# Top-32 attention, gated feed-forward and mixture of experts: the head mask as marks by ScalarE and one GpSimd subtraction, row norm and value product on GpSimd

## What is computed

```
B, H, S, D = 2, 8, 576, 64
scores = q @ k.T / sqrt(D)                       # per head, 576 x 576
keep the 32 largest of each row, the rest -> -1e9
attn = exp(scores - max); attn /= sum + 1e-9
x = (attn @ v) as 1152 rows of 512

xn  = x / sqrt(mean(x*x) + 1e-6) * rms_g
x   = (silu(xn @ w_gate) * (xn @ w_val)) @ w_out     # 512 -> 1536 -> 512

e   = argmax(x @ r_gate), gate = its softmax probability      # 8 experts, room for 288 rows each
out = gate * (relu(x @ w1[e]) @ w2[e])                        # 512 -> 1024 -> 512
```

## Time and profile before

| | |
|---|---|
| median of 3 runs | 741.94 us (741.75 to 743.79) |
| span of the profiled execution, first to last instruction | 741.7 us (the runs list no separate time for it; the median lies 0.2 us above the span) |
| PE busy | 686.1 us, 93% |
| DVE busy | 478.9 us, 65% |
| ACT busy | 270.4 us, 36% |
| POOL busy | 281.5 us, 38% |
| mean granted TensorE clock | 0.948 |

### The profile page before, as it was taken

How to read it: one execution, slowest core, us unless ns; L and a number is a source line. 1 busy time by engine, 2 the same in 40 slices (tenths; PEclk the granted TensorE clock), 3 DMA queues, 4 the chain that set the end, 5 groups by cost and what they waited for, 6 DMA issues and landing times.

```text
span 741.7 us, 10642 instructions
## 1 busy us (share of the span) xinstructions
PE 686.1 (93%) x3862; PEld 557.7 (75%) x3862; DVE 478.9 (65%) x1090; ACT 270.4 (36%) x545; POOL 281.5 (38%) x233
## 2 busy tenths in 40 slices
PE   5696789999999999999999999999994999999994
PEld 3574667588687578688688688687653999999994
DVE  3999979989979968979979979972211011111110
ACT  4385565354354354354354354342210011101110
POOL 1556665646455445545546455452000011110002
PEclk9666599999999999999999999999995999999998
DMA  9999000000000000000000000000055677676501
GB/s 186 363 384 263 0 15 1 0 15 1 14 15 1 15 15 1 11 20 1 14 15 1 15 1 0 15 2 15 0 212 166 256 263 259 231 245 234 204 20 34
DMA packets 52908, 65.43 MB, mean 88 GB/s; under 512 B 32058, under 2 KB 32058, under 8 KB 52860
## 3 DMA queue, kind: packets, MB, share of 16 engines
q1 hardware_dynamic: 51116, 60.05, 25.3%
q0 software_dynamic: 1744, 4.76, 1.7%
HBM read 52.89 MB, written 12.30 MB: 88 GB/s over the span
## 4 chain that ended last, share of the span: by engine, by line
PE 81%; DVE 13%; ACT 1%; DMA 1%; issue 1%; POOL 1%; SPq 0%; POOLq 0%; DVEq 0%; ACTq 0%
PE ps L451 13%; PE ps L593 10%; PE ps L607 10%; PE ps L423 10%; PE ps L401 8%; PE ps L440 6%; PE ps L444 6%; PE ps L441 6%; PE ps L414 4%; PE ps L388 3%; DVE w_top L1006 3%; DVE m L1001 3%; DVE w_parts L909 2%; DVE w_top L993 2%; DVE m L982 1%
## 5 line engine op out<-in xcount | busy, mean ns | idle before, releaser
L1116 POOL TENSOR_SCALAR s_ring<-s_ring,m 128x576 f32<-128x576 f32 x72 | 124.3, 1727 | 179.4 <-DVE m L1010 148.2
L423 PEld LDWEIGHTS ps<-arena,pt_ring 128*128 128x128 f32 (+3 forms) x800 | 99.9, 187 | 22.9 <-issue 8.9
L423 PE MATMUL ps<-arena,pt_ring 128*128 128x65 f32 (+3 forms) x800 | 107.6, 274 | 3.8 <-ACT pt_ring L666 3.7
L1006 DVE MATCH_REPLACE8 w_top<-m,w_top 128x576 f32<-128x576 f32 x144 | 105.8, 742 | 0.0
L1118 POOL TENSOR_TENSOR p_ring<-p_ring,s_ring 128x576 f32<-128x576 f32 x72 | 102.0, 1417 | 6.0
L1001 DVE MAX8 m<-w_top 128x8 f32<-128x576 f32 x144 | 101.6, 747 | 0.0
L451 PE MATMUL ps<-wo_space,hid 128*128 128x512 f32 x216 | 95.8, 593 | 0.0
L401 PE MATMUL ps<-arena,q_cols 128*128 128x288 f32 (+1 forms) x320 | 92.4, 444 | 2.1 <-ACT q_cols L666 1.4
L440 PE MATMUL ps<-w_parts,x_hi 128*128 128x512 f32 x216 | 92.3, 428 | 0.9 <-ACT x_hi L666 0.8
L666 ACT ACTIVATE pt_ring<-ps 128x512 f32<-128x512 f32 (+1 forms) x144 | 54.0, 428 | 95.9 <-PE ps L415 95.6
L441 PE MATMUL ps<-w_parts,x_hi 128*128 128x512 f32 x216 | 85.2, 395 | 0.0
(11 more groups left out here) (116 smaller groups left out, 812.1 us busy)
## 6 DMA issues: line engine op xcount, KB each, us to landing
w_loads<-in_moe_w SPq DMA_DIRECT2D x16, 2048.0 KB, 9.0
dispatched_rows<-hid SPq DMA_DIRECT2D x18, 260.0 KB, 7.4
w_loads<-in_moe_w_gate SPq DMA_DIRECT2D x1, 3072.0 KB, 10.8
w_loads<-in_moe_w_val SPq DMA_DIRECT2D x1, 3072.0 KB, 18.6
wo_space<-in_moe_w_out SPq DMA_DIRECT2D x1, 3072.0 KB, 13.6
arena<-dispatched_rows SPq DMA_DIRECT2D x8, 341.2 KB
out_rows<-hid SPq DMA_DIRECT2D x9, 256.0 KB, 5.2
q_space<-in_q SPq DMA_DIRECT2D x8, 256.0 KB, 2.9
```

Source lines behind the costliest of these rows:

```text
L423: last = mm(ao_ps(u % H, r0, r1), pt_ring[0:n, u % 2, j * P + r0:j * P + r1], vs[b][0:n, j, u % H, :], start=(j == 0), stop=(j == KC - 1))
L1006: vec.match_replace(w_top[:, a, :], m8[:, u % 8, i, :], w_top[:, a, :], NEG).then_inc(s["top_step"], 1)
L1116: gp.tensor_scalar(sc, sc, m8[:, n % 8, TOPK // 8 - 1, 7:8], None, ALU.is_ge).then_inc(s["pchain"], 1)
```

## The change

- The mask. Scale is now in `q_cols` (ScalarE, exact power of two). VectorE writes no bias after the first `max`; at the end of a pair it writes `far`, threshold times 2^90, for both heads. ScalarE makes `relu(far - 2^90 * score)` in `p_ring` (a mark: 0 where the score is kept, huge elsewhere), for both heads of a pair in step u+3 of the even one. GpSimd writes the bias and subtracts the marks from the scores, one operation in place of two. ScalarE's Exp works in place in its step u+4, ahead of `turned_probs`.
- The row norm goes to GpSimd's step B, in front of the rms factor (division as a power of -1).
- The product with the value block goes to GpSimd, which can't read PSUM: ScalarE copies the block, scaled, to `xrow` (`value_rows`, its step B+3+2i), and GpSimd multiplies in its own step B+3+2i.
- The weight split goes to GpSimd for all 12 pieces: two scalings and one subtraction each.

```
-EXP_LAG = 2
+FAR = 2.0 ** 90
-VEC_PIECES = (1, 3, 5, 7, 9, 11)
+VEC_XLO, VEC_SILU, VEC_LOGITS, VEC_RANK, POOL_NORM, POOL_GATED = 2, 2, 12, 16, 0, 3
...
# tensor: value block and turn
-                        pe.wait_ge(s["val_done"], t * 3 + i)
+                        pe.wait_ge(s["val_copied"], t * 3 + i)
                         ffn_block(t, (wv_hi, wv_lo), i, blk[1])
                         turn_hidden(t, i - 1)
...
# scalar
+            def value_rows(tt, i):
+                act.wait_ge(s["blk_full"], tt * 6 + 2 * i + 2)
+                if i == 0:
+                    act.wait_ge(s["t_full"], use["xn", tt] + 1)
+                else:
+                    act.wait_ge(s["val_done"], tt * 3 + i)
+                nc.scalar.activation(xrow[:], blk[1], ACT.Copy, scale=rinv[:, 1:2]).then_inc(s["val_copied"], 1)
...
                 u = n - LAG
+                if 0 <= u < NT * H:
+                    act.wait_ge(s["lowered"], u + 1)
+                    act.wait_ge(s["bias_set"], u // 2 + 1)
+                    nc.scalar.activation(p_ring[:, u % PR, :], p_ring[:, u % PR, :], ACT.Exp,
+                                         bias=nbias[:, u % 8:u % 8 + 1]).then_inc(s["masked"], 1)
                 if 0 <= u < NT * H and u % H > 0:
                     turned_probs(u)
                 if n < NT * H:
                     act.wait_ge(s["s_done"], n + 1)
                     if n >= SR:
-                        act.wait_ge(s["masked"], n - SR + 1)
+                        act.wait_ge(s["lowered"], n - SR + 1)
...
-                u = n - EXP_LAG
-                if 0 <= u < NT * H:
-                    act.wait_ge(s["bias_set"], u + 1)
-                    if u >= PR:
-                        act.wait_ge(s["pt_done"], u - PR + 1)
-                    nc.scalar.activation(p_ring[:, u % PR, :], s_ring[:, u % SR, :], ACT.Exp,
-                                         bias=nbias[:, u % 8:u % 8 + 1], scale=SCALE).then_inc(s["exp_done"], 1)
+                for u in (n - 3, n - 2) if n % 2 else ():
+                    if 0 <= u < NT * H:
+                        act.wait_ge(s["far_set"], u // 2 + 1)
+                        if u >= PR:
+                            act.wait_ge(s["pt_done"], u - PR + 1)
+                        nc.scalar.activation(p_ring[:, u % PR, :], s_ring[:, u % SR, :], ACT.Relu, scale=-FAR,
+                                             bias=far[:, u % 2:u % 2 + 1]).then_inc(s["marked"], 1)
...
# vector: gated(), the odd pieces, the norm and the bias are gone; behind each pair
+                dve.wait_ge(s["th_set"], u0 + 2)
+                if u0 > 0:
+                    dve.wait_ge(s["marked"], u0)
+                vec.tensor_scalar(far[:]..., m8[:, u0 % 8:u0 % 8 + 2, TOPK // 8 - 1, 7:8], FAR, None,
+                                  ALU.mult).then_inc(s["far_set"], 1)
...
# gpsimd, in step n, in this order (behind the scatter of due(n, 16))
+                t = due(n, POOL_NORM)
+                if t is not None:
+                    pool.wait_ge(s["ao_copied"], t + 1)
+                    gp.tensor_scalar(rden[:], ao[:, :, D], EPS_SUM, None, ALU.add).then_inc(s["den_step"], 1)
+                    pool.wait_ge(s["den_step"], 2 * t + 1)
+                    gp.tensor_tensor(rden[:], rden[:], nones[:], ALU.pow).then_inc(s["den_step"], 1)
+                    pool.wait_ge(s["den_step"], 2 * t + 2)
+                    if t > 0:
+                        pool.wait_ge(s["val_done"], t * 3)
+                    gp.tensor_tensor(xrow[:]..., ao[:, :, 0:D], rden[:]..., ALU.mult).then_inc(s["normed"], 1)
                     pool.wait_ge(s["x_sum"], t + 1)          # and the rms factor, as before
...
+                for i in range(FB):
+                    t = due(n, POOL_GATED + 2 * i)
+                    if t is not None:
+                        hb = hid[:, i * 512:(i + 1) * 512]
+                        pool.wait_ge(s["silu_done"], t * 3 + i + 1)
+                        pool.wait_ge(s["val_copied"], t * 3 + i + 1)
+                        gp.tensor_tensor(hb, xrow[:], hb, ALU.mult).then_inc(s["val_done"], 1)
                 m = n - SPLIT_AT
-                if 0 <= m < 4 * FB and m not in VEC_PIECES:
-                    pool.wait_ge(s["w_scaled"], 2 * (m - in_vec(m)) + 2)
+                if 0 <= m < 4 * FB:
+                    pool.wait_ge(s["w_hi_set"], 2 * m + 2)
                     raw, hi, lo, half, cols = split_piece(m)
+                    for c in half:
+                        gp.tensor_scalar(raw[:, c, cols], raw[:, c, cols], gain[:, c:c + 1], None, ALU.mult).then_inc(s["w_scaled"], 1)
+                    pool.wait_ge(s["w_scaled"], 2 * m + 2)
                     gp.tensor_tensor(lo[...], raw[...], hi[...], ALU.subtract).then_inc(s["w_lo_set"], 1)
+                if n < NT * H and n % 2 == 0:
+                    pool.wait_ge(s["th_set"], n + 2)
+                    gp.tensor_scalar(nbias[:, n % 8:n % 8 + 2]..., m8[:, n % 8:n % 8 + 2, 0, 0:1], -1.0, None,
+                                     ALU.mult).then_inc(s["bias_set"], 1)
                 if n < NT * H:
-                    pool.wait_ge(s["th_set"], n + 1)
-                    pool.wait_ge(s["exp_done"], n + 1)
-                    sc, pr = s_ring[:, n % SR, :], p_ring[:, n % PR, :]
-                    gp.tensor_scalar(sc, sc, m8[:, n % 8, TOPK // 8 - 1, 7:8], None, ALU.is_ge).then_inc(s["pchain"], 1)
-                    pool.wait_ge(s["pchain"], 4 + n + 1)
-                    gp.tensor_tensor(pr, pr, sc, ALU.mult).then_inc(s["masked"], 1)
+                    pr = p_ring[:, n % PR, :]
+                    pool.wait_ge(s["marked"], n + 1)
+                    gp.tensor_tensor(pr, s_ring[:, n % SR, :], pr, ALU.subtract).then_inc(s["lowered"], 1)
```

More of the change, by code:

```diff
@@ L9 @@
+import math
 from contextlib import ExitStack
@@ L70, in build @@
     assert B == 2 and NT == 9 and MIX == 4 and H == 8 and KL == 64 and 0 < REST <= P
-    assert S % 2 == 0 and FB == 3 and CF == 12 and CD == 4 and C1 == 8
+    assert S % 2 == 0 and math.frexp(SCALE)[0] == 0.5 and FB == 3 and CF == 12 and CD == 4 and C1 == 8
     disp = nc.dram_tensor("dispatched_rows", [TRASH + N, ROW], F32).ap()
@@ L111, in build @@
         nbias = sb("nbias", [P, 8])
+        far = sb("far", [P, 2])
         rden = sb("rden", [P, H])
@@ L190, in build @@
             "disp_zero out_zero id_set z_set pchain achain vchain "
[L192 removed]
+            "k_turned k_acted k_veced k1_copied w_hi_set w_scaled w_lo_set "
             "t_full t_free "
[L196 to L198 removed]
+            "s_done s_copied top_step th_set far_set bias_set marked lowered masked pt_done pt_copied pv_done "
+            "ao_copied den_step normed x_sum pstep rinv_set x_hi_set blk_full tanh_done silu_done val_copied val_done out_full out_copied "
             "lneg_set lexp_set row_ready seen_set dispatched last_dispatched most_set "
@@ L233, in kind_of @@
             return "mix" if t == MIX else 0 if t < MIX else 1
-        def in_vec(m):
-            return sum(p < m for p in VEC_PIECES)
         def split_piece(m):
@@ L695, in q_columns @@
                 pairs = q_cols[:].rearrange("p (g a) n -> p g a n", a=2)
-                copy(pairs[0:64, :, 0, :], turned[0:64]).then_inc(s["achain"], 1)
+                nc.scalar.activation(pairs[0:64, :, 0, :], turned[0:64], ACT.Copy, scale=SCALE).then_inc(s["achain"], 1)
                 act.wait_ge(s["achain"], t + 1)
-                copy(pairs[64:P, :, 1, :], turned[64:P]).then_inc(s["t_free"], 1)
+                nc.scalar.activation(pairs[64:P, :, 1, :], turned[64:P], ACT.Copy, scale=SCALE).then_inc(s["t_free"], 1)
             def hidden_columns(n):
@@ L810, in _ @@
                         nc.scalar.activation(hi[:, c, cols], raw[:, c, cols], ACT.Copy, scale=gain[:, c:c + 1]).then_inc(s["w_hi_set"], 1)
[L811 to L814, removed]
                 dense(n)
@@ L892, in silu @@
                 vec.scalar_tensor_tensor(out=hb, in0=hb, scalar=1.0, in1=blk[0], op0=ALU.add, op1=ALU.mult).then_inc(s["silu_done"], 1)
[L894 to L898, removed]
-            def beside(n):
[L903 to L910, removed]
+            def beside(n):
                 t = due(n, VEC_XLO)
@@ L952, in beside @@
                     dve.wait_ge(s["row_ready"], t + 1)
[L953 to L962, removed]
-                    vec.tensor_tensor(xrow[:].rearrange("p (h d) -> p h d", h=H), ao[:, :, 0:D],
-                                      rden[:].rearrange("p (h a) -> p h a", a=1).broadcast_to([P, H, D]),
-                                      ALU.mult).then_inc(s["normed"], 1)
             for n in range(0, STEPS, 2):
@@ L985, in _ @@
                     dve.wait_ge(s["top_step"], done + a + 1)
-                    vec.tensor_scalar(nbias[:, u % 8:u % 8 + 1], m8[:, u % 8, 0, 0:1], -SCALE, None,
-                                      ALU.mult).then_inc(s["bias_set"], 1)
-                for a in range(2):
-                    u = u0 + a
                     if u >= 2:
```

(13 more changed lines are left out.)

16 lines of the change are left out of this document (7 added, 9 removed).

## The result

The changed kernel takes 864.72 us (863.76 to 866.55, 4 runs) against 741.85 us (741.72 to 743.79, 4 runs) of the kernel before beside it: ratio 1.1646, 95% interval 1.1621 to 1.1671. Forecast were 856 us, its own range 825 to 880. The profiled execution's span is 864.8 us.

The account below looks back on a forecast made before the run. TensorE, full after the start, was taken to bound the kernel, VectorE only the start. Span 741.7 + start 24 + middle 77.2 + clock 12.6 = 855.5, so 856 us; own range 825 to 880, 8 in 10: 805 to 893.

Parts of the forecast that it names:

- The turn behind GpSimd's queue: Middle: TensorE's turn waits for GpSimd's late product; 30.8 us for block 2, 13.0 for block 0, 11.1 for block 1.
- rival A: Products come in time and only the Exp's later position costs: 774 to 788 us; chance 0.08.
- The Exp's place: Middle: Exp behind ScalarE's dense work delays TensorE's transposes: 11.9, 5.2, 3.1 and 2.1 us, by what stands ahead.
- The clock: Middle: TensorE's clock falls after each of seven 4.4 us holes, 1.8 us each, 12.6 us in all.
- rival C: TensorE's clock falls at the 1.7 us holes as well, 1.8 us each: 892 us; chance 0.07.
- The start: Up to tile 0's first output product: GpSimd's twelve weight pieces, 5.8 us each, set the pace; +24 us.
- step 20: Its first output product, in tile 0, ends the start; predicted near 157 us in place of 133.00.
- the 842 us: Total if GpSimd's weight scalings ran near the lower bound of 0.5 us, as the skill page suggests, in place of 1.54.
- The norm in the middle: Row norm on GpSimd: ready near 371.5 us, wanted at 372 plus a 4.4 us shift, so hidden.
- Relu without a table load: ScalarE's Relu for the marks was claimed to need no table load; the trace has one load in all.
- ScalarE's marks and value copies in idle time: Two marks in place of two Exps, and value copies of 0.7 us, were claimed to fill ScalarE's idle half.
- nothing behind step 76: From tile 7's output products on, norm and product are covered and the experts untouched: 0 us.

Follow-up runs that it names:

- the filled hole: Changed kernel plus four superfluous TensorE products ahead of the turn of block 2 in tiles 0 to 6: 847.34 us; with eight such products, 867.35 us.

## Why the prediction held, point by point

**The turn behind GpSimd's queue (30.8, 13.0 and 11.1 us, together 54.9).** Right in place, number and nearly in size: seven waits of 4.12 us (predicted 4.4), thirteen of mostly 1.38 (1.6), 46.5 us in the middle. The product earlier by a place removed 68.5 us of the middle, where the three terms and the clock make 67.5. That GpSimd is half idle, which spoke for rival A, did not help; that run took no work off GpSimd and got the time back. As idle time alone the 20 waits of the middle are 46.5 us; about 17 more were the clock, and what the 5 left are no run isolates (lost overlap at 0.12 us a wait would be half of them, an estimate).

**The Exp's place (22.3 us).** Right. The middle kept 22.2 us without the product's waits and 21.5 with the mask alone; moving Exp gave 25.3. After gate block 0 TensorE waited 1.55 us (predicted 1.7). The parts overlap a little: in the middle product and Exp moved alone give 68.5 and 25.3, so 93.8, and together with the pieces 86.5.

**The clock (12.6 us).** The mechanism was right, the term too small. At the hole of tile 4 the output products took 7.99 us instead of 7.03, at others up to 9.46; seven of these rows sum to 60.97 against 49.2. With the turn at 1.1 for 0.6, that is 15 us, and the filled hole says 17. By it each hole cost 2.4 us beyond itself. The term that was too small is the 1.8 us of each hole, taken from the transposes and scores at 86.72. After the 1.4 to 1.6 us holes the granted clock stayed at 1.00 (2.4 GHz) in the windows 421 to 427 and 469 to 475 us, so rival C is out; the filled run gives 1.00 over the whole middle although such holes stay in it.

**The start (+24).** The mechanism was right, the size 7 us too small. The scalings on GpSimd took 1562 ns (taken: 1.54 us), a piece 5.5 us (5.8). The queue from the first piece to the last was 102.7 us, of which 12.7 were waits where 7 had been put: 4.95, 2.60 and 1.42 us for marks, which are later because nothing hides their way, and 3.72 for ScalarE's sum of squares behind the norm; and it began 2.3 us later than taken. The last piece ended at 155.0, not 150, and step 20 followed 9 us later, not 7, since the value block ran at the low level (granted clock 0.52 from 155 to 160 us, 5.0 us for 2.9). By undoing in turn: 13 us are the pieces, 9 the places of product and Exp in tile 0, and of the 8.75 left 7.5 are the mask's longer way, by the run with the mask alone. This last term was missing in the prediction; it said that VectorE is not late in the middle, and did not ask it of the start. Missing too was that the norm stands in GpSimd's full queue there: norm and rms factor counted as 3.8 us of work, and undoing the norm gave 10.8. GPSIMD Engine Reference of the Trainium skill (Engine selection) would have one-input operations at roughly line rate. The trace does not agree: the scaling is 3.05 ns an element of the row, more than the 2.46 of the two-input subtraction (1416 ns at 576) on the same engine and over twice the 1.3 of VectorE's `max` over 576. So the measurement decides, and the 842 us that would follow are not seen.

**Hidden terms.** The norm in the middle: right (456.35 for 462.38). Its power of -1 on 128x8 took 1.67 us, twice what both small operations were given, and it fits all the same. Relu without a table load, ScalarE's marks and value copies in idle time, nothing behind step 76 (+1.4): right.

Against the span the sum was 9.3 us short (855.5 for 864.8): 7.0 at the start, 1.4 in the tail, and 0.9 in the middle, where the clock's 4 to 5 more stand against waits some 3 to 4 below their terms. So the middle's 90.7 us against 89.8 is closer than its terms were: two misses of opposite sign nearly cancel there. What is not settled is how the start's 18 us beyond the pieces divide exactly: undone or kept alone, the norm gives 10.6 of the start, the places of product and Exp 9, the mask's way 7.5, so these overlap by about 9; no run takes the norm back together with the pieces.

## What to carry to other kernels

Before moving work to an idle engine, ask not whether it has time but what stands ahead of the work in that engine's queue and which event that waits for: here one place in GpSimd's queue was worth 68 us at a load of 32%. A step number names a place in each queue, and an operation placed behind the work on the newest head is as late as that head. Where a cover is missing (the start, before the dense work is there), cost the same chain again, for a way that is hidden later is bare there; and when several parts are moved, look at each alone, because what paid in the end was one of them, weight pieces off VectorE, in another form than the change's: with ScalarE scaling and the last one kept on VectorE, 1.1% below the kernel before.

## What the runs showed of the hardware

- A hole of TensorE of 4.1 us cost more than itself: the sixteen matmuls behind it took 7.99 to 9.46 us in place of 7.03 (at tile 4 the granted clock was 0.83 from 450 to 460 us), and 3.4 us of useless products in each such hole made the kernel 17.4 us faster. Holes of 1.4 to 1.6 us cost nothing of this kind.
- VectorE and GpSimd take longer for the weights when both work on them at once. The trace of the kernel before has it side by side: VectorE's pair of L909 for one piece takes 3.52 us beside GpSimd's subtraction, and 1.40 us where GpSimd is idle; that subtraction takes 2.84 us beside the pair, and 2.37 at 96.86 us, where no pair of L909 runs.

```profile
49.86 3.52 DVE L909 SCALAR_TENSOR_TENSOR w_parts<-w_loads,gain,w_parts 128x512 fp32r<-128x512 f32 x2
...
90.85 1.40 DVE L909 SCALAR_TENSOR_TENSOR w_parts<-w_loads,gain,w_parts 128x512 fp32r<-128x512 f32 x2
```

```profile
49.98 2.84 POOL L1109 TENSOR_TENSOR w_parts<-w_loads,w_parts 128x1024 fp32r<-128x1024 f32 x1
...
96.86 2.37 POOL L1109 TENSOR_TENSOR w_parts<-w_loads,w_parts 128x1024 fp32r<-128x1024 f32 x1
```

  With only piece 11 on VectorE the group of L909 has a mean of 946 ns for the 1598 with all odd pieces there, beside GpSimd's comparison, which took 2.25 us for its usual 1.73:

```profile
L909 DVE SCALAR_TENSOR_TENSOR w_parts<-w_loads,gain,w_parts 128x512 fp32r<-128x512 f32 x2 | 1.8, 946 | 0.0
```

  And GpSimd's subtraction of 128x1024 has a mean of 2366 ns after the change against 2684 before. What resource the two meet on was not isolated.
- GpSimd's power operation is slow for its size: 1674 ns for 128x8, where adding a constant to 128x8 takes 254.
